# Low-order weights of 64 features as two 64-row matmuls, one in each row half of the array, in a fused two-layer FFN

## The reference, cut to what matters

```python
# x: 2 x 4096 x 192, weight: 8 heads x 7 taps
w = softmax(weight)                       # over the 7 taps
a = causal 7-tap filter of x with w       # 24 features a head; a: 8192 x 192
gate = 1.0 / (1.0 + np.exp(-(a @ moe_w_gate)))      # 192 x 1536
y = (gate * (a @ moe_w_val)) @ moe_w_out            # 1536 x 192
h = y @ moe2_w_in                                   # 192 x 2048
out = np.where(h > 0, h, np.exp(np.minimum(h, 0)) - 1) @ moe2_w_out   # 2048 x 192
```

## Time and profile before

| | |
|---|---|
| time, median of 2 runs | 1299.37 us (1298.86 to 1299.88) |
| span of the profiled execution | 1296.93 us |
| median less that span | 2.44 us |
| PE busy, share of the span | 1273.4 us, 98% |
| PEld busy | 1022.6 us, 79% |
| DVE busy | 920.9 us, 71% |
| ACT busy | 604.6 us, 47% |
| POOL busy | 98.5 us, 8% |
| matmuls, and weight loads | 5440 of each |
| mean granted TensorE clock | 1.000 |

### The profile page before, as it was taken

How to read it: one execution, slowest core, us unless ns; L and a number is a source line. 1 busy time by engine, 2 the same in 40 slices (tenths; PEclk the granted TensorE clock), 3 DMA queues, 4 the chain that set the end, 5 groups by cost and what they waited for, 6 DMA issues and landing times.

```text
span 1296.9 us, 16688 instructions
## 1 busy us (share of the span) xinstructions
PE 1273.4 (98%) x5440; PEld 1022.6 (79%) x5440; DVE 920.9 (71%) x1499; ACT 604.6 (47%) x1053; POOL 98.5 (8%) x88
## 2 busy tenths in 40 slices
PE   4999999999999999999999999999999999999998
PEld 3778888888888888888888888888888888888886
DVE  6987677676776767667676776767767677676776
ACT  4545445354453544545445353544535445354454
POOL 4651000000000000000000000000000000000000
PEclk9999999999999999999999999999999999999999
DMA  4310000000000000000000000000000000000000
GB/s 143 104 50 18 13 16 0 12 16 12 16 0 20 8 12 16 0 28 0 12 16 9 19 0 12 16 12 16 0 12 16 12 16 0 14 14 12 1 13 13
DMA packets 10223, 23.50 MB, mean 18 GB/s; under 512 B 1376, under 2 KB 3424, under 8 KB 10208
## 3 DMA queue, kind: packets, MB, share of 16 engines
q1 hardware_dynamic: 10208, 23.32, 5.8%
HBM read 17.02 MB, written 6.29 MB: 18 GB/s over the span
## 4 chain that ended last, share of the span: by engine, by line
PE 97%; DVE 1%; DMA 0%; POOL 0%; ACT 0%; issue 0%; SPq 0%; DVEq 0%; ACTq 0%
PE hid L188 57%; PE z_acc_a L188 13%; PE y_acc_a L188 11%; PE z_acc_b L188 9%; PE y_acc_b L188 7%; DVE mixed L408 1%; DMA x_in<-x_windows 0%; DMA raw_e<-e_weights 0%; POOL ew L534 0%; DVE xs L417 0%; POOL gw L525 0%; POOL ew L532 0%; DVE ys L417 0%; DVE mixed L405 0%; DVE hidden L478 0%
## 5 line engine op out<-in xcount | busy, mean ns | idle before, releaser
L298 ACT ACTIVATE curve<-hid 128x512 f32<-128x512 f32 x448 | 267.7, 598 | 643.5 <-PE hid L188 643.0
L188 PE MATMUL hid<-xs,gw 128*128 128x512 f32 x1800 | 449.2, 395 | 1.3 <-DVE xs L417 1.3
L188 PEld LDWEIGHTS hid<-xs,gw 128*128 128x128 f32 x1800 | 337.8, 188 | 83.7 <-DVE xs L417 1.7
L188 PE MATMUL hid<-ys,ew 128*128 128x512 f32 x1200 | 318.8, 395 | 0.0
L422 DVE TENSOR_TENSOR h_split<-hidden,h_split 128x512 fp32r<-128x512 f32 x448 | 313.1, 699 | 0.1
L456 DVE TENSOR_TENSOR hidden<-hid,curve 128x512 f32<-128x512 f32 x192 | 132.6, 690 | 210.1 <-ACT curve L298 209.9
L303 ACT CAST h_split<-hidden 128x512 fp32r<-128x512 f32 x448 | 274.3, 612 | 4.7 <-DVE hidden L478 4.7
L188 PEld LDWEIGHTS hid<-ys,ew 128*128 128x128 f32 x1200 | 225.2, 188 | 54.8
L475 DVE TENSOR_SCALAR below<-curve 128x512 f32<-128x512 f32 x256 | 114.9, 449 | 145.1 <-ACT curve L298 145.0
L188 PE MATMUL z_acc_a<-h_split,ew 128*128 128x512 f32 x720 | 206.8, 395 | 0.0
L478 DVE SCALAR_TENSOR_TENSOR hidden<-hid,below 128x512 f32<-128x512 f32 x256 | 177.1, 692 | 8.8
(11 more groups left out here) (52 smaller groups left out, 332.1 us busy)
## 6 DMA issues: line engine op xcount, KB each, us to landing
x_in<-x_windows SPq DMA_DIRECT2D x17, 518.0 KB, 3.2
raw_g<-g_weights SPq DMA_DIRECT2D x12, 352.0 KB, 3.6
out<-z_out SPq DMA_DIRECT2D x16, 256.0 KB, 2.0
raw_e<-e_weights SPq DMA_DIRECT2D x16, 224.0 KB, 2.5
out<-z_out SPq DMA_DIRECT2D x16, 128.0 KB, 2.3
cw<-conv_w SPq DMA_DIRECT2D x1, 7.0 KB, 1.6
```

The lines of the kernel that those rows point to most:

```text
L188: last = nc.tensor.matmul(acc[:], stationary, moving, start=start and n == 0, stop=stop and n == len(pairs) - 1)
L298: nc.scalar.activation(curve[:, t % 2], source[:], func).then_inc(curve_done, 1)
```

## The change

The two low-weight matmuls of a G tile's b features (one for the gate, one for the value, 128 rows each) become two matmuls of 64 rows. The gate's takes rows 0 to 63: low weights on that half, and the high part of the b features. The value's takes rows 64 to 127, where `inp[:, 2]` holds the low part; so the high part is copied once more, to rows 64 to 127 of a new slot `inp[:, 3]`, by a third copy of ACT in `split_x`, for each block. The two high-weight matmuls of the b features now stand together ahead of the pair, in place of one ahead of each low-weight one. PE waits for the new copy through a new semaphore, `x_twin`, ahead of the first tile's pair. The product of low weights by low features, which the 128-row matmuls gave beside, is gone for the b features of G. E phases are as before, through `b_features`.

```diff
-        xs = sb("xs", [P, 3, T], F32R)
-        ys = sb("ys", [P, 3, T], F32R)
+        xs = sb("xs", [P, 4, T], F32R)
+        ys = sb("ys", [P, 4, T], F32R)
...
+        x_twin = sem("x_twin")
...
+            def low_pair(gate, val, t, inp):
+
+                nc.tensor.matmul(gate[:], lo(gw, t, 2)[0:B_ROWS], inp[0:B_ROWS, 2], start=False, stop=True)
+                return nc.tensor.matmul(val[:], lo(gw, t, 3)[B_ROWS:P], inp[B_ROWS:P, 3], start=False, stop=True)
+
...
                     if t == 0:
                         pe.wait_ge(x_ready, 2 * n + 2)
-                    b_features(gate, gw, t, 2, inp)
-                    b_features(val, gw, t, 3, inp).then_inc(hid_done, 1)
+                    nc.tensor.matmul(gate[:], hi(gw, t, 2), inp[:, 2], start=False, stop=False)
+                    nc.tensor.matmul(val[:], hi(gw, t, 3), inp[:, 2], start=False, stop=False)
+                    if t == 0:
+                        pe.wait_ge(x_twin, n + 1)
+                    low_pair(gate, val, t, inp).then_inc(hid_done, 1)
...
                 nc.scalar.copy(inp[:, 2], mixed[:, 1]).then_inc(x_hi, 1)
+                nc.scalar.copy(inp[B_ROWS:P, 3], mixed[B_ROWS:P, 1]).then_inc(x_twin, 1)
```

## The result

The changed kernel takes 1328.49 us (median of 2 runs, 1328.44 to 1328.53) against 1299.37 us: 1.0231 times the time before, 95% interval 1.0215 to 1.0248. The forecast was 1276.0 us, with a range of 1253 to 1320.

The account below looks back on a forecast made before the run. It took PE, busy 98% of the span, as the bound: matmuls times a pitch of 233 ns. The pair's -23.8 us plus 0.4 us of waits gave -23.4 us, so 1276.0 us, range 1253 to 1320.

Parts of the forecast that it names:

- (c) to (e): The new matmul order, ACT's 16 added copies and PE's wait for `x_twin`: each claimed to cost 0.
- (f) and (g): PE's waits growing because it arrives earlier, 0.4 us; DVE and ACT still fitting in a shorter G tile, 0.
- (b): The added 64-row pair in each G tile: 0.343 us in place of 0.467, saving 23.8 us over 192 tiles.
- Full overlap: Rival: both halves of a G tile's pair stream within one pitch, saving 0.233 us a tile, 1255.3 us; chance 0.29.
- the dearest branch of a rival: Emptying at both sides of the G tile's pair plus two exposed loads: +305 ns a tile, 58.6 us, 1358.0 us.
- The rival of emptying: Array empties at each row-count change around the pair: 1316.9 us, or 1337.8 with in-order loads; chance 0.23.

Follow-up runs that it names:

- full rows again: The changed kernel with both low-weight matmuls back at 128 rows, the new order, ACT's third copy and its wait kept: 1298.36 us.
- the two kernels that became faster: The changed kernel with two G tiles' pairs side by side, 1292.09 us; that one with E-phase low-weight b-feature matmuls as 64-row pairs too, 1286.20 us.
- the pair twice: The changed kernel with the 64-row pair issued twice in a row: 1372.82 us, ratio 1.0573.

## Why the prediction was wrong

The parts around the pair held. That PE and its pitch set the time, the 192 tiles and the pitch of 233 ns (behind the slow start) stand, and the moved matmul, ACT's copy and the new wait, (c) to (e), together cost nothing (full rows again, ratio 1.0, interval 0.9991 to 1.001). Terms (f) and (g) are for a PE that arrives earlier, and the changed kernel did not put them to the test; in the two kernels that became faster PE's waits did not grow. That interval also shows that the 2% which I took for the least that a measurement can tell was far too wide.

The step that failed is (b), the cost of the pair: "I take this one because rows 5, 7 and 8 are the only ones that show when a load is issued, and because it also lies midway". It gave 0.343 us for the pair, and the pair with its two sides costs 0.467 + 0.155 = 0.622. It was wrong twice. Inside the pair it was too dear: the second half does not begin 0.11 us behind the first but with it, and a load for the other half passes a waiting matmul (the pair twice). Full overlap, my first rival, was right about the inside. At the sides it was too cheap: it put the changes of row count at 0, and allowed 60 ns each in its own range, where each costs 0.19 us. (That range was wrongly summed as well: on 0.343 us for the pair two switches of 60 ns add 23.0 us, to 1299 us and not to 1288.) 0.107 of that was in my own rows: the price "of a load nobody hides". I had it only in the dearest branch of a rival, and did not ask what hides the load of a 64-row matmul at the only place where it stands, behind a 128-row one.

The rival of emptying was the right mechanism, with its place and its two prices, but no branch of it was the measured one. The dearest, emptying and open loads, came to +305 ns a tile and 1358.0 us; measured is +155. The term that was mis-sized is the emptying: 395 - 233 = 162 ns, the tail of a record under the next one, against 85 to 90 ns. A matmul's end in the record is modelled, and the array takes the next load 0.32 us behind a matmul's beginning, not 0.395. With 87 in place of 162 that branch gives 2 x (87 + 107) - 233 = +155 ns and 1299.4 + 29.8 = 1329.2 us, within the interval of the measured time. The condition that I set for full overlap, a loss where a switch costs over 116 ns, was right: it costs 194. I drew the upper end at 1320 by leaving this branch out, with 0.11 for a loss of over 2%.

The two rules of the Trainium skill that were weighed both hold here. The Trainium skill's page "TensorE: Matmul & The Clock Gate", Part 3, has packed matmuls start some 4 ns apart: the trace agrees, both begin at 644.05, and over the steady part of the trace the mean distance is 3 ns. Between the halves a load also goes out ahead of a waiting matmul (654.99, the pair twice); across the change of row count it does not, and the first load comes after 0.36 us of idle. The Trainium skill's page "TensorEngine Tiling (Array Packing)", Key Properties, has a change of mode drain TensorE but not a change of tile: the trace agrees, at 0.19 us a change, and without one between the two halves. The one says what the inside of a pack gives, the other what its edges take. I weighed them as rivals of each other, and they are terms of one sum.

What stays open: how the 85 to 90 ns come about, and whether other row counts or other widths pay the same. No run varied that. The traces show when the next load goes out; that the array empties until then is the reading of it, not a thing that they record.

## What to carry to other kernels

On a TensorE that runs without a gap, a small-row pack among full matmuls has to earn its edges. Here two changes of row count cost 0.39 us, and a pair of halves earns one pitch, 0.233 us, so one pair loses and two neighbouring pairs win a little. Count changes of row count, not packed matmuls, and gather the packed ones: since sums may be opened by any product, the next tile's can stand beside this tile's without delaying either.

When a mechanism is in doubt, ask of each thing that is hidden now (a load, a tail) whether it would still be hidden, and put the price of its loss into the sum before choosing a middle.

## What the runs showed of the hardware

- A change between 128 and 64 rows costs 0.194 us, the mean of both ways (four of them a tile: 148.9 us over 192 tiles), of which 0.107 is a weight load that did not go out under the matmul ahead.
- The two row halves load at the same time: two loads begin at 654.99 and both their matmuls begin at 655.21 and 655.22; a half alone costs as much as the pair (1328.54 against 1328.49 us).
- Two 64-row matmuls in the same half follow each other like full ones, with the load hidden (0.232 us a tile over the pair in two halves).
- Behind the first 26.1 us the matmuls kept the pitch of 0.233 us between changes of row count, at a granted clock of 1.00, the upper level; gaps of 0.36 us between loads did not lower it. Ahead of that they start 427 ns apart, although the row of the granted clock reads full there too.
